# The first round of token routing: columns compared by GpSimd beside the last attention steps, the others shared by VectorE and GpSimd

## What is computed

```python
logits = x @ w_gate                      # 1536 tokens, 8 experts, 192 places each
order = np.argsort(-logits.flatten())
for idx in order:
    tok, e = idx // E, idx % E
    if assigned[tok] >= 0 or counts[e] >= cap:
        continue
    assigned[tok] = e
    counts[e] += 1
```

## Time and profile before

| what | value |
|---|---|
| runs | 656.37, 656.85, 658.04 us; median 656.85 |
| profiled execution, its own time | 656.8 us |
| its span | 655.1 us |
| TensorE, VectorE, ScalarE, GpSimd busy | 630.3, 420.1, 299.6, 197.7 us |
| mean granted clock of TensorE | 0.994 |
| attention | about 0 to 113 |
| first round, comparisons | 115.6 to 132.2 |
| first expert's matmuls begin | 150.7 |

### The profile page before, as it was taken

One profiled execution on the slowest core, in us unless ns is written; L12 is line 12 of the kernel. 1 busy time (PEld: TensorE's weight loads), 2 busy tenths in 40 slices (PEclk: granted clock), 3 DMA queues, 4 the chain that ended last, 5 costly groups with the idle time before them and its releaser, 6 DMA issues.

```text
span 655.1 us, 12913 instructions
## 1 busy us (share of the span) xinstructions
PE 630.3 (96%) x4964; PEld 557.6 (85%) x4964; DVE 420.1 (64%) x1147; ACT 299.6 (46%) x704; POOL 197.7 (30%) x210
## 2 busy tenths in 40 slices
PE   7799999889999999999999999999999999999995
PEld 4688898558979998889998888899999889999994
DVE  8688887977567778945559798447587420035551
ACT  5778783111122665532326555312365642346652
POOL 5888870010001342221113421211124410123222
PEclk9999999989999999999999999999999999999998
DMA  8377755443260234016203410370035700000001
GB/s 256 142 258 262 262 186 181 158 154 131 103 228 2 89 114 129 2 50 219 111 1 130 138 64 2 105 274 2 1 130 182 247 29 25 1 0 2 1 1 49
DMA packets 31286, 72.37 MB, mean 110 GB/s; under 512 B 2941, under 2 KB 3001, under 8 KB 31225
## 3 DMA queue, kind: packets, MB, share of 16 engines
q1 hardware_dynamic: 27232, 60.69, 26.8%
q0 software_dynamic: 2048, 6.29, 3.3%
q10 hardware_dynamic: 1944, 4.56, 2.1%
HBM read 65.22 MB, written 6.32 MB: 109 GB/s over the span
## 4 chain that ended last, share of the span: by engine, by line
PE 81%; DVE 5%; ACT 1%; POOL 1%; DMA 1%; issue 0%; POOLq 0%; ACTq 0%; DVEq 0%
PE bank L1495 21%; PE bank L1506 20%; PE bank L1408 13%; PE bank L1399 13%; PE bank L1323 3%; DVE beats L882 3%; PE bank L1242 2%; PE bank L1206 1%; PE bank L1188 1%; PE bank L1377 1%; PE bank L1355 1%; PE bank L1263 1%; PE bank L1304 1%; PE bank L1170 1%; DVE ties L891 1%; DMA x_g<-x_rows,tok_next 1%
## 5 line engine op out<-in xcount | busy, mean ns | idle before, releaser
L559 POOL TENSOR_TENSOR wi_lo<-w_in,wi_hi 128x512 fp32r<-128x512 f32 x64 | 85.9, 1346 | 278.6 <-ACT wi_hi L685 278.6
L882 DVE TENSOR_SCALAR beats<-rank_row,key 128x512 bf16<-128x512 f32 (+11 forms) x173 | 107.1, 642 | 18.4 <-PE bank L1325 18.4
L1506 PE MATMUL bank<-wo_hi,g_lo 128*128 128x512 f32 x192 | 76.0, 396 | 0.0
L1506 PE MATMUL bank<-wo_lo,g_hi 128*128 128x512 f32 x192 | 75.7, 394 | 0.0
L1506 PE MATMUL bank<-wo_hi,g_hi 128*128 128x512 f32 x192 | 75.4, 393 | 0.0
L1152 DVE SCALAR_TENSOR_TENSOR g<-bank,g_neg 128x384 f32<-128x384 f32 x64 | 35.5, 554 | 57.9 <-ACT g_neg L738 57.6
L736 ACT ACTIVATE g_neg<-bank 128x384 f32<-128x384 f32 x64 | 31.4, 491 | 78.9 <-PE bank L1495 78.9
L1495 PE MATMUL bank<-y_hi,wi_hi 128*128 128x384 f32 x256 | 58.5, 350 | 0.3 <-DVE g L1152 0.3
L619 ACT ACTIVATE prob<-neg_s,neg_max 128x260 f32<-128x260 f32 x96 | 48.9, 511 | 18.8 <-DVE neg_max L795 17.4
L711 ACT ACTIVATE h_t<-bank 128x192 f32<-128x192 f32 x64 | 21.1, 330 | 77.6 <-PE bank L1399 75.7
L1495 PE MATMUL bank<-y_hi,wi_lo 128*128 128x384 f32 x256 | 55.3, 337 | 0.0
(11 more groups left out here) (163 smaller groups left out, 1377.2 us busy)
## 6 DMA issues: line engine op xcount, KB each, us to landing
w_a<-moe_w SPq DMA_DIRECT2D x8, 1024.0 KB, 7.3
w_a<-moe_w SPq DMA_DIRECT2D x4, 2048.0 KB, 8.9
w_b<-moe_w SPq DMA_DIRECT2D x8, 1024.0 KB, 5.1
w_b<-moe_w SPq DMA_DIRECT2D x4, 2048.0 KB, 8.8
k_raw<-k_t SPq DMA_DIRECT2D x11, 512.0 KB, 4.9
q_raw<-q_t SPq DMA_DIRECT2D x11, 512.0 KB, 4.0
w_in<-moe_w_in SPq DMA_DIRECT2D x8, 512.0 KB, 5.1
w_out<-moe_w_out SPq DMA_DIRECT2D x8, 512.0 KB, 5.5
```

The source lines that it names most:

```text
L559: nc.gpsimd.tensor_tensor(out=wi_lo[:, f % 2, :, :], in0=w_in[:, :, f * P:(f + 1) * P], in1=wi_hi[:, f % 2, :, :].bitcast(F32), op=ALU.sub ...
L882: return nc.vector.tensor_scalar(out=beats[:, c % 3, lo:hi], in0=rank_row[:, lo:hi], scalar1=key[:, c:c + 1], scalar2=None, op0=op)
L1506: last = nc.tensor.matmul(DOWN_BANK[t][:, :], a[:, f % 3, t * P:(t + 1) * P], w[:, f % 2, :], start=(f == 0 and n == 0), stop=(f == FC - 1 ...
```

## The change

OLD = 4 splits the tiles: blocks 0 to 3 of both batches are the 8 old tiles (0 to 3, 6 to 9), blocks 4 and 5 the 4 new ones (4, 5, 10, 11).

- `wanted_key` and `wanted` can now handle a range of blocks. The keys of the old tiles are made in slot 10, behind head 1's maximum, and their wanted experts in slot 13.
- SyncE stores the old keys to DRAM, two copies of 128 x 4 single values, and loads them back as rows broadcast to all partitions, `rank_old`, [128, 1024]. Both stand in its queue at t = 10, around the load of v, with a wait each.
- GpSimd compares the old columns with the old rows as soon as these are there: per column an equality with the column's own tile, the comparison in one or two pieces (`runs`), and a select that keeps the ties in front (`affine_select`). Then, once the new keys are in `rank_row`, it compares three of the four new columns with all 12 tiles.
- VectorE (`compare_rest`) compares the 8 old columns with the new tiles and the first new column with all, and reads the rows from PSUM. TensorE makes the old rows in PSUM too, `old_rows(0)` in slot 13 and `old_rows(1)` behind attention, and the new rows twice: bank 0 for VectorE, bank 4 for ScalarE to copy.
- TensorE's counts follow: `count_old` (8 columns, no zero matmuls between them), `count_rest` (8, two zero matmuls each), `count_new` (4, three each), then four more.
- The last step's sink packing moves from GpSimd to ScalarE.
- The buffers of these values share memory with tensors that are used before or after them (`in_turn`): `beats_old` with `w1_a`, `beats_new` with `h_t`, `rank_old` with `v_sink`, `ties_old` with two masks.

The round's `ties_new` has memory of its own. Rounds 2 to 8 are unchanged. The diff, cut to its core:

```diff
 PAIRS = 4
...
+        OLD_TILES = [b * QB + i for b in range(B) for i in range(OLD)]
+        NEW_TILES = [b * QB + i for b in range(B) for i in range(OLD, QB)]
...
+        NEW_ROWS, OLD_ROWS, ROWS_TO_COPY = bank[0], bank[1:3], bank[4]
+        FIRST_BEATS = B * OLD + 1
...
+        def runs(c, tiles):
+            sides = [t >= c for t in tiles]
+            cuts = [0] + [n for n in range(1, len(tiles)) if sides[n] != sides[n - 1]] + [len(tiles)]
+            return [(lo, hi, ALU.is_le if sides[lo] else ALU.is_lt) for lo, hi in zip(cuts, cuts[1:])]
...
                 if t >= 3:
                     store_x(t - 3)
+                if t == 2 * OLD + 2:
+                    sp.wait_ge(old_keys, 1)
+                    for b in range(B):
+                        tiles = slice(b * QB, b * QB + OLD)
+                        sp.dma_start(key_dram[tiles, :].rearrange("i p -> p i"), key[:, tiles], allow_slow_non_contiguous=True)\
+                          .then_inc(old_keys_stored, 16)
                 if 2 <= t < STEPS:
                     load_v(t)
+                if t == 2 * OLD + 2:
+                    sp.wait_ge(old_keys_stored, 16 * B)
+                    for b in range(B):
+                        sp.dma_start(rank_old[:, b * OLD * P:(b + 1) * OLD * P].rearrange("p (t n) -> p t n", n=P),
+                                     key_dram[b * QB:b * QB + OLD, :].unsqueeze(0).to_broadcast([P, OLD, P]))\
+                          .then_inc(old_rows_loaded, 16)
                 if t >= 3:
                     load_big(t - 3)
...
                 mid, nxt = s - 1, s + 1
-                if 0 <= mid < STEPS:
+                if 0 <= mid < STEPS - 1:
...
-            for s in range(STEPS + 1):
+            for s in range(STEPS):
                 attention_slot(s)
+            def compare_tile(out, row, c, tiles):
+                for lo, hi, op in runs(c, tiles):
+                    nc.gpsimd.tensor_scalar(out=out[:, lo * P:hi * P], in0=row[:, lo * P:hi * P], scalar1=key[:, c:c + 1],
+                                            scalar2=None, op0=op)
+            def equal_keys(out, row, c):
+                nc.gpsimd.tensor_scalar(out=out, in0=row, scalar1=key[:, c:c + 1], scalar2=-1.0,
+                                        op0=ALU.is_equal, op1=ALU.mult).then_inc(equal_found, 1)
+            def only_in_front(out, n):
+                pool.wait_ge(equal_found, n)
+                return nc.gpsimd.affine_select(out=out, in_=out, pattern=[[-1, P]], compare_op=ALU.is_gt, fill=0.0,
+                                               base=0, channel_multiplier=1)
+            pool.wait_ge(consts_ready, CONSTS)
+            pool.wait_ge(old_rows_loaded, 16 * B)
+            for n, c in enumerate(OLD_TILES):
+                equal_keys(ties_old[:, n, :], rank_old[:, n * P:(n + 1) * P], c)
+                compare_tile(beats_old[:, n, :, :].rearrange("p t n -> p (t n)"), rank_old, c, OLD_TILES)
+                only_in_front(ties_old[:, n, :], n + 1).then_inc(old_beats, 1)
+            pool.wait_ge(key_ready, 1)
+            pool.wait_ge(row_copied, 1)
+            for n, c in enumerate(NEW_TILES):
+                if n == 0:
+                    continue
+                equal_keys(ties_new[:, n, :], rank_row[:, n * P:(n + 1) * P], c)
+                compare_tile(beats_new[:, n, 0:B * OLD * P], rank_old, c, OLD_TILES)
+                compare_tile(beats_new[:, n, B * OLD * P:N], rank_row, c, NEW_TILES)
+                only_in_front(ties_new[:, n, :], len(OLD_TILES) + n).then_inc(new_beats, 1)
...
+                    if h == 0 and mid == STEPS - 1:
+                        act.wait_ge(exped, H * STEPS)
+                        act.wait_ge(st_done, mid)
+                        for part in range(3):
+                            last = nc.scalar.copy(sink_p[:, part, :, :], prob[mid % 2][:, :, 2 * P:KW])
+                        last.then_inc(sink_packed, 1)
...
-            for r in range(2):
-                for c in range(3):
-                    copy_row(r, c)
+            act.wait_ge(row_done, 1)
+            nc.scalar.copy(rank_row[:, 0:512], ROWS_TO_COPY[:, :]).then_inc(row_copied, 1)
+            for c in range(3):
+                if c == 0:
+                    act.wait_ge(new_beats, B * (QB - OLD) - 1)
+                copy_row(1, c)
...
+            def wanted_key(r, i=None, ready=key_ready):
+                chain.after(nc.vector.tensor_tensor(
...
+                    if h == 1 and late == 2 * OLD - 1:
+                        dve.wait_ge(consts_ready, CONSTS)
+                        dve.wait_ge(x_ready, 2 * OLD)
+                        wanted_key(0, slice(0, OLD), old_keys)
+                    if h == 3 and s == STEPS + 1:
+                        wanted(0, slice(0, OLD), old_wanted)
...
+            def compare_rest():
+                dve.wait_ge(new_row_done, 1)
+                for n, c in enumerate(OLD_TILES):
+                    at = n * len(NEW_TILES) * P
+                    compare_tile(beats[:, :, :].rearrange("p c n -> p (c n)")[:, at:at + len(NEW_TILES) * P], NEW_ROWS, c, NEW_TILES)\
+                        .then_inc(beats_ready, 1)
+                c = NEW_TILES[0]
+                dve.wait_ge(old_rows_done, B)
+                nc.vector.scalar_tensor_tensor(out=ties_new[:, 0, :], in0=NEW_ROWS[:, 0:P], scalar=key[:, c:c + 1],
+                                               in1=tri_after[:, :], op0=ALU.is_equal, op1=ALU.mult)
+                for b in range(B):
+                    compare_tile(beats_new[:, 0, b * OLD * P:(b + 1) * OLD * P], OLD_ROWS[b], c, OLD_TILES[b * OLD:(b + 1) * OLD])
+                compare_tile(beats_new[:, 0, B * OLD * P:N], NEW_ROWS, c, NEW_TILES).then_inc(beats_ready, 1)
...
-            wanted_key(0)
-            wanted(0)
-            compare_all(0)
+            wanted_key(0, slice(OLD, QB))
+            wanted(0, slice(OLD, QB))
+            compare_rest()
...
+            def old_rows(b):
+                pe.wait_ge(old_keys, 1)
+                pe.wait_ge(maxed, H * STEPS)
+                rows(OLD_ROWS[b], OLD_TILES[b * OLD:(b + 1) * OLD]).then_inc(old_rows_done, 1)
...
+                    if h == 3 and end == STEPS - 1:
+                        old_rows(0)
...
+            def count_old(n):
+                c = OLD_TILES[n]
+                if n == 0:
+                    pe.wait_ge(old_wanted, 1)
+                    pe.wait_ge(halves_read, STEPS)
+                    nc.tensor.matmul(COUNTS, ones_row[:, :], start_row[:, :, :], start=True, stop=False, skip_group_check=True)
+                pe.wait_ge(old_beats, n + 1)
+                count_tiles(beats_old[:, n, :, :].rearrange("p t n -> p (t n)"), OLD_TILES, c)
+                count_ties(ties_old[:, n, :], c, False)
+            def count_rest(n):
+                c, at = OLD_TILES[n], n * len(NEW_TILES) * P
+                pe.wait_ge(beats_ready, n + 1)
+                count_tiles(beats[:, :, :].rearrange("p c n -> p (c n)")[:, at:at + len(NEW_TILES) * P], NEW_TILES[:-1], c)
+                t = NEW_TILES[-1]
+                nc.tensor.matmul(COUNTS[:, t, :], beats[:, :, :].rearrange("p c n -> p (c n)")[:, at + 3 * P:at + 4 * P], want[:, c, :],
+                                 start=False, stop=False, skip_group_check=True).then_inc(counted, 1)
+            def count_new(n):
+                c = NEW_TILES[n]
+                if n == 0:
+                    pe.wait_ge(want_ready, 1)
+                    pe.wait_ge(beats_ready, FIRST_BEATS)
+                else:
+                    pe.wait_ge(new_beats, n)
+                count_tiles(beats_new[:, n, :], OLD_TILES + NEW_TILES, c)
+                count_ties(ties_new[:, n, :], c, n == len(NEW_TILES) - 1).then_inc(counted, 1)
...
+            old_rows(1)
             keep_clock(6, spare)
-            for c in range(3):
-                rows(0, c)
-            keep_clock(5, spare)
-            for c in range(NT):
-                count(0, c)
-                keep_clock(3 if c < NT - 1 else 8, spare)
+            pe.wait_ge(key_ready, 1)
+            rows(NEW_ROWS, NEW_TILES).then_inc(new_row_done, 1)
+            rows(ROWS_TO_COPY, NEW_TILES).then_inc(row_done, 1)
+            for n in range(len(OLD_TILES)):
+                count_old(n)
+            for n in range(len(OLD_TILES)):
+                count_rest(n)
+                keep_clock(2, spare)
+            for n in (1, 0, 2, 3):
+                count_new(n)
+                keep_clock(3, spare)
+            keep_clock(4, spare)
             across(0)
             keep_clock(1, spare)
...
+            pe.wait_ge(key_ready, 2)
+            pe.wait_ge(row_copied, 1)
             for c in range(3):
-                rows(1, c)
+                rows(ROW_BANK[c], range(4 * c, 4 * c + 4)).then_inc(row_done, 1)
```

120 lines of the change are left out of this document (78 added, 42 removed).

## The result

| | before | changed |
|---|---|---|
| median of the runs | 657.4 us (656.4 to 658.3, 4 runs) | 685.8 us (684.8 to 689.0, 4 runs) |
| the profiled execution, its span | 656.8 us, 655.1 us | 689.0 us, 686.9 us |
| last count of the first round | 132.7 us | 162.4 us |
| first matmul of the first expert | 150.7 us | 182.7 us |

The ratio is 1.044, with a 95% interval from 1.040 to 1.048: 28.4 us more by the medians. The forecast was 649.6 us, with a range up to 659.5. It was wrong in its sign and in its range.

What follows compares the result with a forecast made beforehand. The prediction took VectorE to bound the first round's comparisons. The last count was to move from 132.70 to 125.7, plus 0.2 for one zero matmul fewer: 7.2 us off 656.8, forecast 649.6 us, range 647.0 to 659.5.

Steps and rivals of the forecast that it cites:

- GpSimd's price: GpSimd's compares in the first round: 0.16 us an instruction and 0.87 ns a column, taken from a copy.
- its other end: GpSimd's compares priced by the subtraction of two tensors, 2.17 ns a column: old part 26.0 us, new part 13.8.
- The rival with GpSimd as the bound: First round: GpSimd ends last once a column costs over 1.51 ns; 666.1 us at the subtraction's price, chance 0.17.
- The store: SyncE's store of the old keys to DRAM in 1024 pieces of 4 bytes, behind slot 10: taken at 4.5 us.
- 99.9: Time in us when GpSimd can start its old part, after the keys' store (4.5) and load (4.2); ends 97.5 and 105.5.
- the pair: Key store and row load on SyncE's queue: holding up later loads costs nothing unless they take over some 10 us.
- Its compares from PSUM: VectorE's remaining compares in the first round: 5.0 us for old columns, 7.1 with the new column, no waiting for GpSimd.
- The chained operations on SBUF: VectorE's small `wanted_key` and `wanted` operations: each waits 0.25 us on average beside GpSimd's instructions.
- steps (1) to (7): Attention from slot 10 to VectorE's new compares: key 1.5 us later, at 115.2, and VectorE's `wanted` done at 117.5.
- steps (1), (3) and (4): Slot 10's added VectorE work, +0.4 us; `old_rows(0)` in slot 13, +0.3; `wanted` on the old half, +0.4.
- The key in slot 10: Rival: its third operation comes second to GpSimd's k subtraction, VectorE stands until 93.2; 1.9 us more, 651.5, chance 0.12.
- Little is left: Rival: key store over 15 us, or TensorE's clock falls while waiting in the old counts; 655 us, chance 0.08.

Runs made afterwards that it cites:

- e5: e2 with GpSimd doing only the old part, VectorE comparing all four new columns from PSUM and TensorE counting the old columns last: 661.2 us, ratio 1.0056.
- e1: The kernel before plus 13 GpSimd instructions run alone behind its last output, to price a compare and its variants: 689.2 us in one run.
- e2: The changed kernel with the old keys turned by TensorE, copied by VectorE and stored as ten whole rows: 678.7 us, ratio 1.034.
- e3: The changed kernel with SyncE's wait for the key store and the load of the rows one turn of its loop later: 687.1 us, ratio 1.046.
- e4: The kernel before with the old keys made in slot 10, stored in small pieces and loaded as rows that nobody reads: 660.8 us, ratio 1.0053.
- e7: e4 without the load of the rows and without SyncE's wait; VectorE waits for the store ahead of the last key: 662.1 us, ratio 1.0069.
- e10: The kernel before with turned store, GpSimd comparing eight old columns with old rows, one zero matmul and not three behind their counts: 660.5 us, ratio 1.0040.
- e6: e2 with matmuls on zeros where TensorE waits for GpSimd's beats: 681.2 us, ratio 1.035.

## Why the prediction was wrong

**The step that failed is GpSimd's price.** "I take the copy's price, because its operands are the compare's." A compare of 1024 columns cost 2.86 us, with nothing beside it as in the kernel; the copy 1.04. With 0.28 us and 2.51 ns a column in the forecast's own formula, 36 instructions, 14208 columns and 11 selects are 10.1 + 35.7 + 3.2 = 49.0 us. Measured are 49.3, where the sum had 21.3 and its other end 39.8. The prediction bounded an operation that it had no row for by two others, and took it that "a second read is the plain difference between the two rows". The runs show that the price goes by the kind of instruction: with a scalar, even a constant one, it is 2.77 us and more for 1024 columns, and a second tensor in the scalar's place brings it down to 1.90. "Over 1.51 ns a column" GpSimd was the bound by the prediction itself, so this one term turns the sign. The page's rule that was set beside it, 1.69 ns by an estimate (the Trainium skill, GPSIMD Engine Reference, Performance pitfalls for Q7 kernels), had the sign right and 659.2 us; it is low as well, against 2.51 measured. That section is about kernels written for the engine's cores, and this is a built-in instruction; whether that makes the difference no run here shows.

**The rival with GpSimd as the bound was the case**, and its mechanism is confirmed: TensorE counts to the last column and waits for GpSimd, as the chain and e5 show. Its 0.17 was too little. The two ends were used as if the true value had to lie between them, though the text of the rival itself had the reason for a higher one, "a compare must turn a truth value into a number, and its scalar is read per partition". e1 shows that the scalar's column isn't it (3%), and that a multiplication costs the same.

**The store.** Taken at 4.5 us, bounded at 9.9; it took 11.7 from its issue to the load's. The load took 7.8 and not 4.2, 3.3 of it in issuing the two DMAs. "I take 4.5 for the store, since the queue is quiet here" had no row for 1024 pieces either. With e2 this is worth 7.1 us. The forecast's 99.9 is also 0.35 more than the terms it is added up from. The "cost nothing unless the pair takes over some 10 us" of the queue had the condition right: the pair took 19.5, SyncE was held for 15.0 of them, and v and x's buffer were late, but in the changed kernel that cost nothing (e3). The small pieces have a cost of their own, some 4 to 5 us where nothing hides it (e4, e7), for which the prediction has no term.

**VectorE.** Its compares from PSUM took 8.1 us and not 7.1: 5.9 for the 4 instructions of 512 and 8 of 256 columns (5.0 predicted) and 2.3 for the new column (2.1). The prediction charged these nothing for GpSimd, and they show no wait beside it: all eight of 256 columns take 475 ns, and the others 743 to 751. The row that it gave for this, the copy of 0.69 us at 100.84, had nothing beside it: GpSimd has no instruction there between 96.4 and 103.5. The chained operations on SBUF were to wait 0.25 us each; most waited for nothing, a few for 0.2 to 0.8 (the key 0.65 and not 0.17, `want` 0.69). By the Trainium skill (SBUF — State Buffer, Who interferes with whom) the one that comes second stands for the whole of the other's instruction. That some wait and that the reads from PSUM don't is seen here; the whole isn't: in e10 `ties` began at 126.22, inside a GpSimd instruction of 2.69 us that ran until 128.68, and ended at 127.31; the next `ties`, at 127.63, took its usual 0.34 inside the same one. The measurement decides here.

**Attention.** The steps (1) to (7) came to +1.5 us at the key and put VectorE's first new compare at 117.5. With the small pieces gone there is less: in e2 the logits of step 7 are at 89.34 (before: 89.62), the last ones at 112.64 (112.58), the last part of the key at 113.62, and the first new compare at 115.2. So from the logits of step 7 to the last ones the change costs 0.3, where steps (1), (3) and (4) had 1.1, and the waits were nearly all too dear. The key in slot 10 was not caught behind GpSimd: it is made at 90.38 in e2, ahead of GpSimd's subtraction at 90.53, and at 92.98 in the changed kernel, 0.15 ahead of it (93.13), the margin that was called thin.

**Little is left** had its clock: 0.50 and 0.70 in TensorE's waits, and a tail of 20.3 us for 18.0. That is 2.3 of 28, and the zeros that e6 put into the wait didn't buy it back.

By the medians the loss splits into 7.1 us for the store in small pieces (changed kernel to e2), 17.5 for GpSimd's three new columns (e2 to e5), and 4.1 for what e5 still has over the kernel before, its later last count and the low clock behind it. (The sum is 28.7 and not 28.4, because the kernel before was measured anew with them, at 657.2.)

## What to carry to other kernels

An operation that the profile doesn't show isn't bounded by the rows of others; where it is the largest term and the forecast's sign hangs on it, the range has to reach past the dearest row, and one run of that instruction alone settles it. Storing 1024 single values as pieces of 4 bytes cost more here than turning them by TensorE and storing whole rows. Work given to a second engine isn't free because that engine is idle: it counts from the time at which its inputs are there, and what it does to the first engine's instructions has to be taken off the gain.

## What the runs showed of the hardware

- GpSimd's instruction with a scalar costs 0.28 us and 2.51 ns a column, for a compare and a multiplication alike, with bf16 or f32 output; a second operation in it adds 0.85 ns a column. A copy costs 1.04 us and a subtraction of two tensors, one of them a column spread out, 1.90 us for 1024 columns (e1).
- The store of 1024 pieces of 4 bytes took 11.2 us (changed kernel), with the DMA engines 95% busy at 19 GB/s (e7), and a load of v issued behind it landed after 12.6 us and not 2.7. It comes with a stop of 2 to 3 us of TensorE, VectorE, ScalarE and SyncE at once, which the profile puts down to no instruction (e7).
- VectorE's instructions on SBUF lose 0.5 to 0.75 us near each start of a GpSimd instruction on SBUF, 4.7 us over 16 us, and GpSimd loses 2.0 (e10); VectorE's compares from PSUM show none of it (475 ns for 256 columns, each time).
- The executions whose first expert began at a granted clock of 1.00 took 504.1 to 504.4 us from its first matmul to the end of the span; the three where the clock fell to 0.50 there took 506.0 to 506.1 (e3, e5, e10).
